# Block 0's first feed-forward stage: gates and values regrouped, four banks in turn, follow-up work behind the attention slots

## What is computed

```
attn  = softmax(q k^T / 8, keep: first 4 keys or the last 128) v        # 2 x 8 heads x 768 x 64
x     = attn as (1536, 512)
x     = (silu(x w_gate) * (x w_val)) w_out      # stage B, d_ff 1536, weights 512 x 1536
g     = x w_in2;  g = max(g, 0) + alpha * min(g, 0)
out   = g w_out2                                # stage C, d_ff 2048
```

## Time and profile before

| | |
|---|---|
| median of 3 runs | 657.35 us (657.31 to 657.67) |
| profiled execution | 658.04 us |
| its span, first to last instruction | 656.1 us |
| PE busy | 628.2 us, 96% |
| POOL, DVE, ACT busy | 442.8, 406.5, 260.2 us |
| granted TensorE clock, mean | 0.994 |

### The profile page before, as it was taken

The page is one execution under the profiler, slowest core; times in us unless marked ns, Lnnn a source line. Parts: engine busy times, 40 slices in busy tenths (PEclk is TensorE's granted clock), DMA queues, the critical chain, the costliest instruction groups (busy, mean ns, idle before and its releaser), DMA issues. The chain is left out here.

```text
span 656.1 us, 9469 instructions
## 1 busy us (share of the span) xinstructions
PE 628.2 (96%) x3072; PEld 489.5 (75%) x3072; DVE 406.5 (62%) x696; ACT 260.2 (40%) x597; POOL 442.8 (67%) x592
## 2 busy tenths in 40 slices
PE   8889988999999989999999999997999999999998
PEld 5566766677667768787787878875788888888886
DVE  4954655555567655565656474897667755656474
ACT  4646555574645531211212121434533442325150
POOL 6847778787875879988879675589997875510000
PEclk9999999999999989999999999998999999999999
DMA  9343432311322012121212231002222211000005
GB/s 292 106 145 113 130 109 85 114 50 38 107 83 62 17 34 80 49 64 33 64 33 65 80 82 49 16 1 64 65 64 65 66 32 65 1 0 1 0 4 189
DMA packets 28815, 44.62 MB, mean 68 GB/s; under 512 B 2816, under 2 KB 8960, under 8 KB 28768
## 3 DMA queue, kind: packets, MB, share of 16 engines
q1 hardware_dynamic: 28624, 43.76, 21.8%
q10 hardware_dynamic: 144, 0.26, 0.1%
HBM read 40.87 MB, written 3.15 MB: 67 GB/s over the span
## 5 line engine op out<-in xcount | busy, mean ns | idle before, releaser
L1634 POOL TENSOR_TENSOR w_lo<-raw_weights,w_hi 128x512 fp32r<-128x512 f32 (+1 forms) x124 | 151.6, 1223 | 9.9
L1633 POOL CAST w_hi<-raw_weights 128x512 fp32r<-128x512 f32 (+1 forms) x124 | 74.1, 598 | 45.2 <-PE ffn_ps L1945 18.1
L2286 DVE TENSOR_TENSOR scratch<-ffn_ps,scratch 128x512 f32<-128x512 f32 x112 | 76.4, 687 | 39.0 <-PE ffn_ps L1945 38.4
L1662 POOL TENSOR_TENSOR w_lo<-part_sum,w_hi 128x256 fp32r<-128x256 f32 x80 | 61.2, 766 | 6.4
L1860 PE MATMUL ffn_ps<-x_hi,w_hi 128*128 128x512 f32 x152 | 61.8, 406 | 1.9 <-ACT gate_sb L2045 0.9
L1860 PE MATMUL ffn_ps<-x_hi,w_lo 128*128 128x512 f32 x152 | 59.4, 391 | 0.0
L1860 PE MATMUL ffn_ps<-x_lo,w_hi 128*128 128x512 f32 x152 | 59.2, 390 | 0.0
L1714 POOL TENSOR_TENSOR scratch<-scratch,inv 128x264 f32<-128x264 f32 (+1 forms) x48 | 30.3, 632 | 36.0 <-DVE inv L2159 35.8
L1945 PE MATMUL ffn_ps<-h_hi,w_hi 128*128 128x512 f32 x128 | 51.1, 399 | 2.5 <-DVE scratch L2286 2.5
L1945 PE MATMUL ffn_ps<-h_hi,w_lo 128*128 128x512 f32 x128 | 49.9, 390 | 0.0
L1919 PE MATMUL att_ps<-t_hi,w_hi 128*128 128x512 f32 x112 | 45.4, 405 | 4.7 <-DVE value_sb L2209 3.2
(11 more groups left out here) (207 smaller groups left out, 1577.9 us busy)
## 6 DMA issues: line engine op xcount, KB each, us to landing
raw_weights<-pieces SPq DMA_DIRECT2D x118, 256.0 KB, 2.8
k_sb<-kt SPq DMA_DIRECT2D x12, 264.0 KB, 3.5
v_sb<-vt SPq DMA_DIRECT2D x12, 256.0 KB, 2.7
out<-scratch SPq DMA_DIRECT2D x12, 256.0 KB, 2.0
q_sb<-qt SPq DMA_DIRECT2D x11, 256.0 KB, 3.5
scratch<-vs SPq DMA_DIRECT2D x1, 384.0 KB, 5.7
q_sb<-qt ACTq DMA_DIRECT2D x1, 256.0 KB, 2.7
alpha<-alpha_t SPq DMA_DIRECT2D x1, 8.0 KB, 6.8
```

What stands on the lines that cost most here:

```text
L1633: chain(pool.tensor_copy(hi, raw[:, r % n_raw, at]))
L1634: last = pool.tensor_tensor(lo, raw[:, r % n_raw, at], hi.bitcast(F32), ALU.subtract)
L1662: pool.tensor_tensor(lo, s, hi.bitcast(F32), ALU.subtract).then_inc(split_done, 1)
L2286: ins = dve.tensor_tensor(total, back_ps(key), total, ALU.add)
```

## The change

Fronts of a group are put in another order: the gate products of f = 0 and f = 1, then the two value products. All eight chunks of a group come in one piece, followed by the four backs of the group before. Both SiLUs stand together, behind the second gate product. Each front product and each back of block 0 up to C1 takes the next of the four banks of `ffn_ps` (`in_turn`), and waits for whatever used that bank four uses before (`bank_ahead`, `wait_for_use`). All follow-ups of a chunk (SiLU, product, evacuation, `x2`) now stand behind the slots of that chunk. What was due later (`rest`, `x2_rest`, stage C's rounding) comes one chunk later (`waiting`). In the fill the parts of the sums come in the order T2, T3, T1, T4, spread over more chunks, the last ones among the strips. The stage C sums' parts take the same order at their old places. The loads and POOL's weight jobs follow the order of use.

```diff
@@ -843,7 +843,9 @@
     STRIPS = (("A11", "B11", 0), ("S2", "T2", 1), ("A12", "B21", 0), ("S3", "T3", 1), ("S1", "T1", 2),
               ("A22", "T4", 1), ("S4", "B22", 2))
     N_STRIPS, N_MIXES = len(STRIPS), 5
     T_ORDER = {"B": ("T1", "T3", "T2", "T4"), "C": ("T1", "T2", "T3", "T4")}
+    T_PARTS = ("T2", "T3", "T1", "T4")
     TILE = {(0, 1): 3, (0, 2): 1, (1, 1): 0, (1, 2): 2}
     ROLE = {(0, 1): 0, (1, 1): 1, (0, 2): 2}
@@ -867,8 +869,9 @@
     def slot(w, lo, hi):
         return ("slot", tuple(u if lo <= u < hi else None for u in range(w, w - LAG - 1, -1)))
-    def fronts(g, f):
-        return [("front", (g, f, part, half)) for part in range(parts[g[0]] - 1) for half in range(2)]
+    def fronts(g):
+        return [("front", (g, f, part, half)) for part in range(parts[g[0]] - 1) for f in range(F) for half in range(2)]
     def backs(g):
         return [("back", (g, single, d)) for d in range(4)]
@@ -952,21 +955,20 @@
     part_one = []
     for n, g in enumerate(groups_b):
-        for f in range(F):
-            part_one += fronts(g, f)
-            if f == 0 and n and g != last_b:
-                part_one += backs(groups_b[n - 1])
-    part_one += backs(groups_b[-2]) + backs(last_b)
+        part_one += fronts(g)
+        if n:
+            part_one += backs(groups_b[n - 1])
+    part_one += backs(last_b)
     turn_at = len(part_one) - 1
-    part_one += fronts(groups_c[0], 0) + fronts(groups_c[0], 1)
+    part_one += fronts(groups_c[0])
     next_w = early + 1
     n_spread = n_units + LAG - next_w
     placed = 0
-    low_next = []
+    waiting = [[], []]
     for n, chunk in enumerate(part_one):
         what, key = chunk
+        plan.append(chunk)
         slots_here = []
         while placed < n_spread and (placed + 1) * len(part_one) <= n_spread * (n + 1):
             slots_here.append(slot(next_w, early, n_units))
@@ -974,58 +976,61 @@
         if n == turn_at and not slots_here:
             slots_here.append(slot(next_w, early, n_units))
             placed, next_w = placed + 1, next_w + 1
-        now, later = [], []
+        now, later = waiting
+        waiting = [later, []]
         if what == "back":
-            now = [("evac", key)] + low_next
-            low_next = []
+            now = [("evac", key)] + now
             if key[0] == last_b:
-                now.append(("x2", (single, key[2])))
-                low_next = [("x2_rest", (single, key[2]))]
-                if n == turn_at:
-                    now += low_next
-                    low_next = []
+                now.insert(1, ("x2", (single, key[2])))
+                waiting[0].append(("x2_rest", (single, key[2])))
         elif key[3] == 1:
             h = (key[0], key[1], single)
             if key[0][0] == "C":
-                now, later = [("relu", h)], [("hidden", h), ("rest", h)]
+                now = now + [("relu", h)]
+                waiting[0] += [("hidden", h)]
+                waiting[1] += [("rest", h)]
             elif key[2] == 0:
-                later = [("silu", h)]
+                if key[1] == F - 1:
+                    now = now + [("silu", (key[0], f, single)) for f in range(F)]
             else:
-                now, later = [("hidden", h)], [("rest", h)]
-        plan.append(chunk)
-        plan += now
+                now = now + [("hidden", h)]
+                waiting[0] += [("rest", h)]
+        if n == turn_at:
+            now, waiting[0] = now + waiting[0], []
+        rest = []
         for item in slots_here:
+            plan += rest
             rest = emit_slot(item)
-            plan += later
-            later = rest
-        plan += later
+        plan += rest + now
+    behind += waiting
     def parts_of_sums(stage):
-        steps = []
-        for n in range(4):
-            steps += [[("thi", (stage, n, kk)), ("tlo", (stage, n, kk))] for kk in range(half_k)]
-        return steps
+        return [(stage, name, kk) for name in T_PARTS for kk in range(half_k)]
+    fill = fronts(groups_c[1]) + backs(groups_c[0]) + fronts(groups_c[2]) + backs(groups_c[1]) + strips(pair_b[0], 0)
     steps = parts_of_sums("B")
-    fill = (fronts(groups_c[1], 0) + fronts(groups_c[1], 1) + backs(groups_c[0])
-            + fronts(groups_c[2], 0) + fronts(groups_c[2], 1) + backs(groups_c[1]))
+    low_after = dict(zip((6, 8, 9, 10, 11, 14, 16, 18), steps))
+    high_after = dict(zip((5, 7, 8, 9, 10, 13, 15, 17), steps))
     for n, chunk in enumerate(fill):
         emit_chunk(chunk)
-        if n >= 6 and steps:
-            plan += steps.pop(0)
+        if n in low_after:
+            plan.append(("tlo", low_after[n]))
+        if n in high_after:
+            plan.append(("thi", high_after[n]))
     for n, g in enumerate(pair_b):
         if n == 0:
-            for chunk in strips(g, 0) + backs(groups_c[2]) + strips(g, 1):
+            for chunk in backs(groups_c[2]) + strips(g, 1):
                 emit_chunk(chunk)
         if n + 1 < len(pair_b):
             for chunk in strips(pair_b[n + 1], 0) + pair_backs(g) + strips(pair_b[n + 1], 1):
                 emit_chunk(chunk)
-    steps = parts_of_sums("C")
-    for chunk in fronts(groups_c[3], 0) + fronts(groups_c[3], 1):
+    steps = [[("thi", key), ("tlo", key)] for key in parts_of_sums("C")]
+    for chunk in fronts(groups_c[3]):
         emit_chunk(chunk)
     low_next = None
     for t in pair:
...
@@ -1087,21 +1092,29 @@
             tsum_no["C", n, kk] = len(tsum_no) + 1
-    back_home, back_ahead, had = {}, {}, {}
+    back_home, front_home, bank_ahead, had = {}, {}, {}, {}
     rest_of_b = (2, 3, 4, 0, 1, 4, 0, 1)
-    for key in back_no:
-        g, t, d = key
-        if g[0] == "B" and t != single:
-            home = (rest_of_b if g != pair_b[-1] else (2, 0, 1, 2, 0, 1, 2, 0))[4 * (t - 1) + d]
-        elif g[0] == "C" and (t != single or g[1] > 2):
-            home = len(had.get("all", [])) % 3
-            had.setdefault("all", []).append(key)
-        else:
-            home = back_no[key] % 2
-        back_home[key] = home
+    in_turn = (3, 4, 0, 1)
+    for what, key in chunks:
+        home = None
+        if what == "back":
+            g, t, d = key
+            if g[0] == "B" and t != single:
+                home = (rest_of_b if g != pair_b[-1] else (2, 0, 1, 2, 0, 1, 2, 0))[4 * (t - 1) + d]
+            elif g[0] == "C" and (t != single or g[1] > 2):
+                had["all"] = had.get("all", -1) + 1
+                home = had["all"] % 3
+            elif g == groups_c[2]:
+                home = d % 2
+        elif what == "strip" or key[3] == 1 or (key[0][0] == "C" and key[0][1] > 2):
+            continue
+        if home is None:
+            home = in_turn[(len(front_home) + len(back_home)) % 4]
+        (back_home if what == "back" else front_home)[key[:3]] = home
         if home in had:
-            back_ahead[key] = had[home]
-        had[home] = key
+            bank_ahead[what, key[:3]] = had[home]
+        had[home] = (what, key[:3])
     hs = [key for what, key in plan if what == "hidden"]
     assert hs == [key for what, key in plan if what == "rest"]
     assert list(evac_no.values()) == [back_no[key] for key in evac_no]
@@ -1381,7 +1394,9 @@
             return n - 2 if n <= last else n - 1
         def front_ps(g, f, part):
-            return bank(ffn_ps, part) if g[0] == "B" else bank(att_ps if g == groups_c[3] else ffn_ps, f)
+            if (g, f, part) in front_home:
+                return bank(ffn_ps, (front_home[g, f, part] + 2) % 5)
+            return bank(att_ps if g == groups_c[3] else ffn_ps, f)
         def strip_ps(m, role):
@@ -1823,36 +1838,38 @@
...
+            def wait_for_use(use):
+                what, key = use
+                if what == "back":
+                    pe.wait_ge(evac_done, back_no[key])
+                elif key[0][0] == "B" and key[2] == 0:
+                    pe.wait_ge(silu_done, silu_no[key[0], key[1], single])
+                else:
+                    pe.wait_ge(prod_done, prod_no[key[0], key[1], single])
             def front(g, f, part, half):
                 n = g[1]
                 if half == 0:
                     pe.wait_ge(split_done, job_no["piece", piece_key(g, f, part, single)])
                 if g[0] == "B":
-                    if n == 0 and f == 0 and part == 0:
+                    if n == 0 and part == 0 and f == 0:
                         pe.wait_ge(xlo_done, x_rests_until(quads_t - 1) - (1 if half == 0 else 0))
-                    if half == 0 and (n or f):
-                        ahead = (g, 0, single) if f else (groups_b[n - 1], F - 1, single)
-                        if part == 0:
-                            pe.wait_ge(silu_done, silu_no[ahead])
-                        else:
-                            pe.wait_ge(prod_done, prod_no[ahead])
-                else:
-                    if n == 0 and f == 0:
-                        pe.wait_ge(x2lo_done, x2_no[single, (half + 1) * half_k - 1])
```

(48 more changed lines are left out.)

20 lines of the change are left out of this document (10 added, 10 removed).

## The result

| | before | after |
|---|---|---|
| median, both on the same chip | 657.51 us (657.31 to 660.22) | 647.69 us (647.55 to 649.49) |
| profiled execution, its span | 658.04, 656.1 us | 647.59, 645.9 us |
| mean granted clock | 0.994 | 0.997 |

The ratio is 0.985, with an interval from 0.982 to 0.988: the kernel is 9.8 us faster. Forecast were 648.3 us, in a range from 645.0 to 654.0.

A forecast was written before the change was run, and what follows sets the result against it. TensorE was taken as the bound everywhere. Stalls won 9.4 (part one) + 4.75 (fill) = 14.15 us, new ones 5.1, net 9.05: profiled 658.04 to 649.0, 0.7 above the median, so 648.3 us; range 645.0 to 654.0.

The forecast's parts named there:

- end, new+old: End of part one, where C0 starts: stalls of 0.45 + 1.3 = 1.75 us instead of 0.6.
- Table loads: Part one: pairing the SiLUs removes 12 loads, relieving ACT of 15.4 us, which counts only through the scores' wait.
- The walk through the list: ACT's and DVE's work followed through part one: scores late by 0.7 (B0), 1.15 (B1), 0.45 (B2), 1.05 us (B4).
- The drain of 1.38 us a switch: Skill's rule on ACT's table switches, left out: ACT relieved of 32 us, pairs later, time 653.8.
- four banks in turn: Part one: reusing banks four uses later removes the backs' stalls of 1.64 and 1.20 us and the gate's 1.04.
- the fill: Fill: with four banks a back needs a front's product instead, ready early; worth all 4.75 us and the clock.
- Follow-ups behind the slots: Part one: `rest` queued ahead of the next mask makes scores wait 1.15 us in group B1, 1.05 in B4.
- That part one gives nothing: Rival: in part one the follow-ups behind slots cost as much as the loads gave; 653.75 us, chance 0.22.
- The slower one (659.9): Rival: in part one a mask behind a waiting `rest` costs 1.15 us at all 12 product places; chance 0.06.
- The better one (645.8): Rival: the returned stalls are smaller, likely half, as DVE's or ACT's queue is freer; 645.8 us, chance 0.15.
- That a load stays before each SiLU: Rival: a load stays, or six groups pay 1.28 us more for the pair's first SiLU; 652.2 us, chance 0.04.

The follow-up runs named there:

- after_exp: The changed kernel with Exp in place of SiLU in stage B, so no table loads: 644.52 us, ratio 0.978.
- after_rest_late: The changed kernel with each remainder (`rest`) of stage B's part one one chunk later still: 646.29 us, ratio 0.979.
- before_exp: The kernel before the change with Exp in place of SiLU in stage B, so no table loads there: 648.93 us, ratio 0.984.
- before_newfill: The kernel before the change with only the fill's sums' parts in the new order and places: 653.15 us, ratio 0.990.
- after_oldfill: The changed kernel with the fill's sums' parts in their old order and places: 651.81 us, ratio 0.988.
- Experiments 3 and 4: Changed kernel with each SiLU behind its own gate product: 650.30 us; changed kernel with evacuations, products and x2 ahead of their chunk's slot: 646.52 us.
- after_backpairs: The changed kernel with gates and backs sharing banks 0 and 1, values in 2 and 3: 669.41 us, ratio 1.015.
- after_twobanks: The changed kernel with gates in banks 0 and 1, values and backs sharing 2 and 3, and a changed wait at the first strips: 673.43 us, ratio 1.021.

## Why the prediction was right, and which of its steps were not

**Right in direction, size and place.** The net of 9.05 us stands against the 9.08 of the two stretches, 4.3 against 4.43 in part one and 4.75 against 4.65 in the fill. That the sums agree so closely is in part luck: the terms that came out too large (0.19 us after chunk 6) and the one that was missing (0.34 after 35) nearly cancel, and the booking to causes was wrong in two steps, below. Place by place, what came:

```
after chunk            forecast   measured
6   (B0)                 0.70       0.51
17  (B1)                 1.15       1.20
26  (B2)                 0.45       0.53
35                        -         0.34
53  (B4)                 1.05       1.19
71, 72 (end, new+old)    1.75       1.88
```

**Table loads: right.** 12 loads of 1283 ns went, as counted. What was to be seen with it, four places of waiting scores with 3.3 us, came as five with 3.4. The walk through the list, with the trace's durations, had all four of its places right. The drain of 1.38 us a switch that the prediction cites from the Trainium skill and leaves out, and by which the time would have been 653.8, isn't there: the ACTIVATE at 67.91 starts 1.30 us after its load at 66.61, the six loads ahead of a SiLU have 0.1 us idle before them in all, and ScalarE's busy time fell by 15.3 us for 12 loads.

**A missed term: the stall after chunk 35.** The step took 0.67 to 0.70 us for the remainders. The one in that place took 1.58:

```profile
110.91 1.27 POOL L1649 TENSOR_TENSOR w_lo<-raw_weights,w_hi 128x512 fp32r<-128x512 f32 x1
111.15 1.58 DVE L2208 TENSOR_TENSOR x_lo<-scratch,x_hi 128x512 fp32r<-128x512 f32 x1 [1.91 <-ACT x_hi L2028]
...
113.26 0.16 DVE L2158 COPY_PREDICATED att_ps<-sink_out,masked_score 128x8 f32<-128x8 int32 x1
```

Then came an evacuation and, at 113.26, the mask. The other three of its form took about 0.70. The price of 1.77 for two, named in the prediction, was the hint, but it was misread as 0.9 each: in the trace of before these are 1.17 and 0.68 us, one remainder with a GpSimd subtraction beside it and one without. The stall also moves with GpSimd: counted from the start of chunk 33, GpSimd's normalising (L1729), queued behind a subtraction for weights, starts at 0.32 us in the changed kernel, 0.70 in `after_exp` and 0.90 in `after_rest_late`. The stall is 0.34, 0.74 and 0.93. There TensorE has come ahead of GpSimd's weight work, which is why that stall grows where others go.

**The step "four banks in turn": not the first cause.** It credited the banks with the backs' stalls of 1.64 and 1.20 us and the gate's 1.04. `before_exp` has the old banks and 0.33, nothing and nothing there. The stalls came out of the same queue as the scores': VectorE's product waiting for a SiLU behind a load, with the evacuation behind it. The profile names the last link, the evacuation; who held VectorE up stood one row further back, as in the earlier trace rows, and the step didn't look there for the backs. Half of the loads are still in the changed kernel, though, and no run has the old order with four banks: how much of these 3.9 us the banks would have saved by themselves stays open.

**The step "the fill": the banks weren't needed.** It took the product of the front as new condition "with four banks", and put the 4.75 us there. `before_newfill` gets 4.5 us without the banks, and `after_oldfill` with the banks and the old order keeps a stall of 1.7 us in the fill and one of 1.14 at a strip. Either edit cures the stall after chunk 89; only the order cures all of it. It does so because the two `tlo`s that waited for ACT no longer stand ahead of the evacuation.

**What the banks are for.** With the old order of the sums they bring 2.85 us in the fill, less 1.14 at a strip; with the new one only 0.13 us is left there for them. But the new order of part one needs them: with banks by kind it is 21 to 24 us slower than with four in turn, by the ratios. So the sum came out right although two of its terms were booked to one edit where another, or either, would have done. Undone one at a time, the banks alone lose 20 us, twice the whole gain: what an edit costs to undo is not what it brought.

**Follow-ups behind the slots.** The prediction booked the four waits of the scores to the pairs and to this placement together. Experiments 3 and 4 divide them: single SiLUs cost 1.7 us, and evacuations and products put back ahead save 1.7. What helps is the pair and, as far as the runs tell, the order of the chunks, which puts one or more between a SiLU and its product; that the order does it is argued, since it was never run without the four banks and without stalls of theirs.

**Rivals.** That part one gives nothing would have needed nearly twice the returns that were found; its 653.75 has 1.15 us in it that the text doesn't explain (without them it is 652.6). The slower one (659.9) needed a mask behind a waiting `rest` at ten places by its own sum, not nine, and it was two. The better one (645.8) wanted the new stalls at half their size; they came at 110%. That a load stays before each SiLU falls with the count of 12.

**Open.** What the order of the chunks and what the four banks bring in part one, each without the other. The 0.77 us in stage B's strips, and the start of chunk 0 (41.23 us here, 41.65 before, 41.05 to 42.35 over all profiled executions), differ between executions of one kernel and are not the change's.

## What to carry to other kernels

A wait that the profile gives to VectorE's evacuation may belong to an instruction ahead of it in VectorE's queue that waits for ScalarE; go one row further back before a bank is blamed alone. Fewer switches of ScalarE's tables can pay even where that engine is idle 43% of the time, if an in-order queue stands behind each result. And an instruction that waits for another engine goes behind the next thing that the critical engine needs, not ahead of it: moving `rest` by one chunk took 2 us out of the changed kernel.

## What the runs showed of the hardware

**VectorE's subtractions in SBUF wait for GpSimd's.** The remainder of 1.58 us started at 111.15, while a GpSimd subtraction ran from 110.91 to 112.18, and ended 0.55 us behind it, at 112.73. Another, in the end of part one:

```profile
193.41 1.61 POOL L1649 TENSOR_TENSOR w_lo<-raw_weights,w_hi 128x512 fp32r<-128x512 f32 x1
194.40 1.17 DVE L2326 TENSOR_TENSOR x_lo<-scratch,x_hi 128x512 fp32r<-128x512 f32 x1
```

GpSimd ended at 195.02, VectorE at 195.57, again 0.55 us later. TensorE's first chunk of C0, which needs that remainder, starts at 195.67. The Trainium skill ("SBUF — State Buffer", "SBUF: two separate sides") says that a VectorE instruction with two SBUF inputs and a GpSimd instruction that reads SBUF hold a port pair in turn and each for its whole length; the two rows agree with it, with their 0.55 us behind GpSimd's end, most of the 0.70 us that such a remainder takes by itself. Evacuations, whose one input is in PSUM, took 0.68 us in the same stretch.

**A clock that falls after a stall.** Where `after_backpairs` had TensorE busy for 7.49 of 10 us, the granted clock was 1.00, and in the 10 us behind it 0.83, at 9.52 us busy; the low part is 0.50, the 1.2 GHz level, from 200.9 to 204.3 us, and begins 0.4 us after a wait of 2.14 us has ended. In `after_twobanks` a wait of 4.00 us ended at 78.42, and the clock was 0.50 from 77.5 to 84.3. In the kernel before, the fill had 0.94 with its two stalls, and 0.52 from 231.9 to 235.2, right behind the wait of 2.43 us; with the order of the sums alone changed, it had 1.00. Not every stall is followed by it: the fill of `after_oldfill` has 1.00 with a wait of 1.56 us.
